# Adding the two halves of an attention chunk on VectorE instead of TensorE, with the mask pieces staged by ScalarE

## The chip, the cores and the metric

One core of one Trainium2 chip runs the kernel. The metric is the time of one execution on the device, in microseconds (us). Kernels are compared by the median of several runs; the profile shows one execution.

## What is computed

Attention with a bucket mask, followed by two MoE-like layers. The change touches attention alone. Its reference, cut to what matters (2 batches x 8 heads, 768 rows, head width 64, 6 bits):

```python
q_bits = (np.einsum('bhsd,dk->bhsk', q, proj) > 0)
k_bits = (np.einsum('bhsd,dk->bhsk', k, proj) > 0)
mask = q_bucket[:, :, :, None] == k_bucket[:, :, None, :]   # bucket = the 6 bits as a number
scores = scale * np.matmul(q, k.transpose(0, 1, 3, 2))
scores = np.where(mask, scores, -1000000000.0)
attn = np.exp(scores - max); attn = attn / (sum + 1e-09)
out = np.matmul(attn, v)
```

The result is laid out as 1536 rows of 512 and goes through relu(x w_in)^2 w_out and then through a routed layer of 8 experts.

## The kernel before

The 16 heads are worked in 8 pairs (`pair`, once for the first, a loop over six, once for the last). A pair has 12 tiles of 128 query rows by 768 keys, tt = 0 to 11, six for each head; three tiles make a chunk, so a pair has four chunks c = 0 to 3. Every engine has its own instruction queue, written out by hand in the order given here, and semaphores join them.

TensorE (`pair`, L1419 ff.) does for each tile tt, in this order: the scores of tile tt+2 (`scores`, L1373: four matmuls, 512 and 256 columns of each of two stacked operands; the mask rows are part of the operands); the first three transposes of the probabilities of tile tt (`turn_probs`, L1392, ring of three PSUM units); four products with v (`times_v`, L1406 and L1407, 384 columns each, into the PSUM bank PV); the other three transposes. Where tt-4 is a multiple of 3, all six transposes come ahead of the products, and the products start a new chunk. Beside the scores of tiles 2, 3, 5, 6, 8, 9 (MASK_TILES) a sixth of the next pair's mask is computed (L1324); beside those of tiles 10, 1, 4, 7 (BACK_TILES) a finished chunk is turned back (`turn_back`, L1355).

v is split into a rounded part and its remainder, side by side in 128 columns, so PV holds two halves of 64 partitions whose sum is the chunk's result, turned. ScalarE copies all 128 partitions to oT (`keep_oT`, L687), and TensorE multiplies oT with `fold`, two unit matrices of 64 on top of each other, which adds the halves and turns them back:

```python
for j in range(CHUNK_TILES):
    last_mm = mm(beside(z, CHUNK_TILES * HD)[:, HD * j:HD * j + HD], oT[c % 2][:, P * j:P * j + P],
                 fold, start=True, stop=True)
```

Each of these float32 matmuls shows as two matmul records and two weight loads.

ScalarE does for each tile tt: the exp with its row sums (`exp`, L667, two records), then for tile tt-1 the rounding of two units to pt_hi (`round_units`, L678), and where tt-7 is a multiple of 3 the copy to oT. The first rounding of a chunk and the copy wait for the end of an earlier chunk's products (pv_done).

VectorE does for each tile tt: for tile tt+1 the staging of a mask piece (`stage_mask`, L910 and L912, PSUM to mask_st, only for MASK_TILES), the scaling of a turned chunk into x_rows (`keep_x`, L955, only for BACK_TILES) and the maximum (L930); for tile tt-1 the two remainders pt_lo (`rest_units`, L939, which free a PSUM unit). Pieces 0 to 2 are 1 where the count of equal bits is the full one (popc), pieces 3 to 5 are -BIG where it is less.

GpSimd splits q, k and v of the next pair, and copies mask_st to the stacked operands (`place_masks`, through `copied`, L520). SyncE issues the loads. The waits that matter for the change:

```python
pe.wait_ge(oT_done, i * CHUNKS_PER_PAIR + c)                # times_v, first part of a chunk: PV is free
pe.wait_ge(oT_done, i * CHUNKS_PER_PAIR + (c + 1))          # turn_back
pe.wait_ge(exp_done, i * TILES_PER_PAIR + (tt - 1))         # scores
```

Of the kernel before, what the change touches and what calls it, by code (L numbers as in the profile page):

```python
# [5 lines left out]
F32 = mybir.dt.float32  # L6
# [4 lines left out]
ALU = mybir.AluOpType  # L11
# [57 lines left out]
def program(nc, qT, kT, v, proj_blocks, patterns, w_in, w_out, sb_rows, mod_id, mod_bias, w_gate, w1, w2,  # L69
            consts, tri, out):  # L70
    y_rows = nc.dram_tensor("y_rows", (TOK, DM), F32).ap()
    with ExitStack() as ctx:
# [33 lines left out]
        mb_sb = sb("mb_sb", [P, 2, NE], F32)  # L106
        oT = [sb(f"oT{c}", [P, CHUNK], F32) for c in range(2)]
        row_sum = sb("row_sum", [P, CHUNKS_PER_PAIR, CHUNK_TILES, 2], F32)
        row_eps = sb("row_eps", [P, CHUNKS_PER_PAIR, CHUNK_TILES], F32)
        row_inv = sb("row_inv", [P, CHUNKS_PER_PAIR, CHUNK_TILES], F32)  # L110
        x_rows = sb("x_rows", [P, PAIRS, QT, 2 * HD], F32)
        after_x = place[0]
# [186 lines left out]
        qk_split = sem("qk_split")  # L299
        masks_turned = sem("masks_turned")  # L300
        masks_staged = sem("masks_staged")
        masks_in = sem("masks_in")
# [207 lines left out]
        def _(pool):  # L510
# [33 lines left out]
            def place_masks(i, z):  # L544

                pool.wait_ge(masks_staged, i * MASK_UNITS + MASK_UNITS)
                pool.wait_ge(scores_done, i * TILES_PER_PAIR + (QT * (z + 1) - TILES_PER_PAIR))
                m = half(z, True)
                for c, stack in ((0, qb), (1, kb)):
                    copied(stack[z][m, :], mask_st[m, c, :], 1.0, masks_in, i * 4 + (2 * z + c + 1))  # L550

# [99 lines left out]
        def _(act):  # L651
# [29 lines left out]

            def keep_oT(i, c, first):
                act.wait_ge(pv_done, i * CHUNKS_PER_PAIR + (c + 1))
                if not (first and c < 2):

                    act.wait_ge(x_done, i * CHUNKS_PER_PAIR + (c - 1))
                nc.scalar.activation(oT[c % 2][:, :], ps[:, PV, 0:CHUNK], ACT.Copy).then_inc(oT_done, 1)  # L687

            def pair(i, first, last):
                for tt in range(TILES_PER_PAIR):  # L690
                    exp(i, tt, first)
                    if tt > 0:
                        round_units(i, tt - 1, first)
                    elif not first:
                        round_units(i - 1, TILES_PER_PAIR - 1, False)
                    c, r = divmod(tt - 7, CHUNK_TILES)
                    if r == 0:
                        if c >= 0:
                            keep_oT(i, c, first)
                        elif not first:  # L700
                            keep_oT(i - 1, c + CHUNKS_PER_PAIR, False)

            pair(0, True, False)
            with act.Fori(1, PAIRS - 1) as i:
# [10 lines left out]
            round_units(PAIRS - 1, TILES_PER_PAIR - 1, False)  # L715
            keep_oT(PAIRS - 1, 2, False)
            for t in range(1, 4):
                round_xt(t)
            keep_oT(PAIRS - 1, 3, False)

# [173 lines left out]
        def _(v_):  # L894
            v_.wait_ge(const_in, 16 * 7)
            nc.vector.memset(row_sum[:, :, :, 1], 1e-9).then_inc(eps_known, 1)
            v_.wait_ge(eps_known, 1)
# [7 lines left out]

            def stage_mask(m, part, dst, src):

                col = MASK_W * (m % 3)
                if m < 3:
                    return nc.vector.tensor_scalar(dst[part, col:col + MASK_W], src[part, :], popc[part, :], None,  # L910
                                                   ALU.is_equal)
                return nc.vector.tensor_scalar(dst[part, col:col + MASK_W], src[part, :], popc[part, :], -BIG,  # L912
                                               ALU.is_lt, ALU.mult)

            def tile_max(i, tt, first, last):

                z = tt % 2
                v_.wait_ge(scores_done, i * TILES_PER_PAIR + (tt + 1))
                if tt in MASK_TILES and not last:

                    v_.wait_ge(masks_in, i * 4 + 4)
                    m = MASK_TILES.index(tt)
                    stage_mask(m, slice(0, P), mask_st[:, m // 3, :], beside(z, MASK_W)).then_inc(masks_staged, 1)
                if tt in BACK_TILES:
                    c = BACK_TILES.index(tt)
                    if c == 0:
                        keep_x(i, c, z)
                    elif not first:
                        keep_x(i - 1, c, z)
                nc.vector.tensor_reduce(neg_max[:, z:z + 1], score_bank(z), AX, ALU.max,  # L930
                                        negate=True).then_inc(max_done, 1)

            def rest_units(i, tt):

                c, j = divmod(tt, CHUNK_TILES)
                for h in range(2):
                    v_.wait_ge(hi_done, i * (2 * TILES_PER_PAIR) + (2 * tt + h + 1))
# [22 lines left out]
            def pair(i, first, last_):  # L960
                for tt in range(TILES_PER_PAIR):
# [4 lines left out]
                    if tt > 0:  # L966
                        rest_units(i, tt - 1)
                    elif not first:
                        rest_units(i - 1, TILES_PER_PAIR - 1)

# [14 lines left out]
            for c, stack in ((0, qb), (1, kb)):  # L985
# [3 lines left out]
                for z in range(2):  # L989
                    for m in units:  # L990
                        v_.wait_ge(masks_turned, m + 1)
                        placed = stage_mask(m, half(z, True), stack[z], first_mask(m))
                        if z == 1:
# [24 lines left out]
            last_rows(1)  # L1018
            invert(PAIRS - 1, 3)
            for t in range(1, 4):  # L1020
                rest_xt(t)
            last_rows(2)
            last_rows(3)
# [295 lines left out]
        def _(pe):  # L1319
# [31 lines left out]
            def turn_back(i, c, z):  # L1351

                pe.wait_ge(oT_done, i * CHUNKS_PER_PAIR + (c + 1))
                for j in range(CHUNK_TILES):
                    last_mm = mm(beside(z, CHUNK_TILES * HD)[:, HD * j:HD * j + HD], oT[c % 2][:, P * j:P * j + P],  # L1355
                                 fold, start=True, stop=True)
                return last_mm

            def scores(i, tt, first, last):
# [11 lines left out]
                for a, b, start in ((qa[z], ka[z], True), (qb[z], kb[z], False)):  # L1371
                    for lo, hi in ((0, 512), (512, SEQ)):
                        last_mm = mm(bank[:, lo:hi], a[:, P * j:P * j + P], b[:, lo:hi], start=start, stop=not start)  # L1373
                if tt in MASK_TILES and not last:
# [75 lines left out]

            end = PAIRS - 1
            turn_back(end, 1, 1).then_inc(back_done, 1)
            times_v(end, 2, 2, False)
# [6 lines left out]

            pe.wait_ge(x_done, end * CHUNKS_PER_PAIR + 2)
            turn_back(end, 2, 1).then_inc(back_done, 1)

# [19 lines left out]
            def beside_first_step(f):  # L1483

                if f == 0:

                    pe.wait_ge(x_done, PAIRS * CHUNKS_PER_PAIR - 1)
                    turn_back(PAIRS - 1, 3, 1).then_inc(back_done, 1)
                if f == 1:
# [303 lines left out]
```

## Time and profile before

| | us |
|---|---|
| median of 3 runs | 732.97 (732.0 to 734.8) |
| the profiled execution | 731.03 |
| its span, first to last instruction | 729.2 |
| attention, within the span | to about 266 |
| TensorE busy | 704.5 |
| VectorE busy | 428.0 |
| ScalarE busy | 321.6 |
| GpSimd busy | 266.8 |

The span is what the trace covers; 1.8 us of the execution lie around it. PE is TensorE's matmuls, PEld its weight loads, which run beside the matmuls; DVE is VectorE, ACT ScalarE, POOL GpSimd. Matmuls are pipelined, so durations of neighbours overlap, and the pace of a group is read from the starts. The span divides into projections and first masks (to 33 us), attention, the first layer and the routed layer.

### The profile page before, as it was taken

To read this page: it belongs to the slowest core of one execution; us is meant where nothing else is said; L and a number is where in the kernel's file an instruction comes from. 1 tells how busy PE (TensorE), PEld (TensorE's weight loads), DVE (VectorE), ACT (ScalarE), POOL (GpSimd) and SP (SyncE) were. 2 spreads that over 40 slices of the span, in tenths; PEclk is the share of its full clock that TensorE was granted. 3 is DMA by queue.
4 is the path that set the end of the run, shared out by engine and by line. 5 is a ranking of instruction groups with operands and counts; after the bars stand their busy time and mean duration, and the time that the engine had idled before them with its cause. 6 is when DMAs were issued, how large, how long until landed. Compare 5 with 4: busy or idle time off the path is not lost.

```text
span 729.2 us, 12070 instructions
## 1 busy us (share of the span) xinstructions
PE 704.5 (97%) x3810; PEld 587.8 (81%) x3810; DVE 428.0 (59%) x825; ACT 321.6 (44%) x634; POOL 266.8 (37%) x271
## 2 busy tenths in 40 slices
PE   7799999999999999999999999999999899999994
PEld 3389999999999987888888888888885688877883
DVE  0589999999999956548555643564197611333110
ACT  0078878788787854221222221123144223443221
POOL 0666777677667751007004500720001222121111
PEclk9989999999999999999999999999999999999999
DMA  9921321321233030001100300001135541001011
GB/s 296 264 59 55 105 55 55 97 65 54 80 81 117 1 116 0 1 2 58 58 1 0 115 0 0 1 8 51 58 132 183 190 161 59 29 30 45 32 56 47
DMA packets 22508, 51.32 MB, mean 70 GB/s; under 512 B 3168, under 2 KB 5344, under 8 KB 22464
## 3 DMA queue, kind: packets, MB, share of 16 engines
q1 hardware_dynamic: 19008, 42.34, 18.3%
q0 software_dynamic: 2480, 7.87, 3.3%
q10 hardware_dynamic: 976, 0.56, 0.3%
q8 instruction: 23, 0.38, 0.2%
q14 instruction: 21, 0.17, 0.1%
HBM read 44.47 MB, written 6.55 MB: 70 GB/s over the span
## 4 chain that ended last, share of the span: by engine, by line
PE 89%; DVE 4%; DMA 2%; ACT 1%; issue 1%; SPq 1%; ACTq 0%; POOL 0%; POOLq 0%; DVEq 0%
PE ps L1373 9%; PE ps L1392 9%; PE ps L1576 6%; PE ps L1578 6%; PE ps L1577 6%; PE ps L1540 6%; PE ps L1542 6%; PE ps L1541 6%; PE ps L1406 5%; PE ps L1407 5%; PE ps L1661 3%; PE ps L1663 3%; PE ps L1662 3%; PE ps L1631 3%; PE ps L1633 3%; PE ps L1632 3%
## 5 line engine op out<-in xcount | busy, mean ns | idle before, releaser
L678 ACT ACTIVATE pt_hi<-ps 128x384 fp32r<-128x384 f32 x192 | 88.0, 499 | 42.1 <-PE ps L1392 26.9
L939 DVE TENSOR_TENSOR pt_lo<-ps,pt_hi 128x384 fp32r<-128x384 f32 x192 | 100.1, 551 | 10.4 <-ACT pt_hi L678 6.3
L731 ACT ACTIVATE relu<-ps 128x512 f32<-128x512 f32 x48 | 28.7, 598 | 175.6 <-PE ps L1542 175.6
L667 ACT ACTIVATE probs<-ps,neg_max 128x768 f32<-128x768 f32 x96 | 87.3, 909 | 26.0 <-DVE neg_max L930 25.9
L1392 PE MATMUL ps<-cst,probs 128*128 128x128 f32 x576 | 90.7, 275 | 0.9 <-DVE pt_lo L939 0.9
L930 DVE TENSOR_REDUCE neg_max<-ps 128x1 f32<-128x768 f32 x96 | 90.9, 946 | 0.0
L1117 DVE TENSOR_TENSOR sq<-relu 128x512 f32<-128x512 f32 x48 | 36.4, 759 | 71.6 <-ACT relu L731 71.2
L1540 PE MATMUL ps<-xt_hi,wi_hi 128*128 128x512 f32 x192 | 75.8, 395 | 0.0
L1576 PE MATMUL ps<-wo_hi,g_hi 128*128 128x512 f32 x192 | 74.9, 390 | 0.6 <-DVE xt_lo L1007 0.6
L1392 PEld LDWEIGHTS ps<-cst,probs 128*128 128x128 f32 x576 | 70.6, 145 | 5.9 <-DVE pt_lo L939 1.6
L1542 PE MATMUL ps<-xt_hi,wi_lo 128*128 128x512 f32 x192 | 74.8, 390 | 0.0
L1541 PE MATMUL ps<-xt_lo,wi_hi 128*128 128x512 f32 x192 | 74.7, 389 | 0.0
L1578 PE MATMUL ps<-wo_hi,g_lo 128*128 128x512 f32 x192 | 74.7, 389 | 0.0
L1577 PE MATMUL ps<-wo_lo,g_hi 128*128 128x512 f32 x192 | 74.7, 389 | 0.0
L1406 PE MATMUL ps<-pt_hi,vs 128*128 128x384 f32 x192 | 72.7, 379 | 0.0
L1407 PE MATMUL ps<-pt_lo,vs 128*128 128x384 f32 x192 | 64.7, 337 | 0.0
L520 POOL TENSOR_SCALAR wi_hi<-wi_raw 128x512 fp32r<-128x512 f32 x16 | 10.0, 622 | 143.3 <-PE ps L1542 140.5
L1154 DVE TENSOR_TENSOR y_acc<-ps,y_acc 128x512 f32<-128x512 f32 x48 | 32.4, 691 | 50.1 <-PE ps L1578 50.1
L1373 PE MATMUL ps<-ka,qa 128*128 128x512 f32 x192 | 57.3, 380 | 2.3 <-ACT probs L667 1.2
L1373 PE MATMUL ps<-kb,qb 128*128 128x512 f32 x192 | 50.3, 344 | 0.0
L639 POOL DMA_INDIRECT out<-y_slot,put_now x13 | 13.3, 1023 | 99.6 <-ACT y_slot L826 99.6
L1191 DVE TENSOR_TENSOR hT_lo<-ps,hT_hi 128x512 fp32r<-128x512 f32 x24 | 15.5, 685 | 53.0 <-ACT hT_hi L818 52.9
(198 smaller groups left out, 1473.0 us busy)
## 6 DMA issues: line engine op xcount, KB each, us to landing
w_raw<-w SPq DMA_DIRECT2D x16, 512.0 KB, 6.8
raw_k<-kT SPq DMA_DIRECT2D x32, 192.0 KB, 3.3
raw_q<-qT SPq DMA_DIRECT2D x32, 192.0 KB, 3.6
wi_raw<-w_in SPq DMA_DIRECT2D x4, 1024.0 KB, 5.1
wo_raw<-w_out SPq DMA_DIRECT2D x4, 1024.0 KB, 5.1
pair_raw<-qT SPq DMA_DIRECT2D x8, 384.0 KB, 6.7
pair_raw<-kT SPq DMA_DIRECT2D x8, 384.0 KB, 13.6
raw_v<-v SPq DMA_DIRECT2D x16, 192.0 KB, 2.4
```

The costliest lines, as they stand in the source:

```text
L930: nc.vector.tensor_reduce(neg_max[:, z:z + 1], score_bank(z), AX, ALU.max, negate=True).then_inc(max_done, 1)
L939: nc.vector.tensor_tensor(pt_lo[c % 2][sl], unit(tt, h).rearrange("p (k q) -> p k q", k=3), pt_hi[c % 2][sl].bitcast(F32), ALU.subtract).t ...
L1373: last_mm = mm(bank[:, lo:hi], a[:, P * j:P * j + P], b[:, lo:hi], start=start, stop=not start)
L1392: last_mm = nc.tensor.transpose(unit(tt, h)[:, P * u:P * u + P], probs[tt % 2][:, P * kt:P * kt + P], ident)
L1406: mm(ps[:, PV, 0:CHUNK], vs[z][:, kt, :], pt_hi[c % 2][:, kt, :], start=(kt == 0), stop=False)
L1407: last_mm = mm(ps[:, PV, 0:CHUNK], vs[z][:, kt, :], pt_lo[c % 2][:, kt, :], start=False, stop=(kt == QT - 1))
L1540: mm(ps[:, f, :], wi_hi[:, k, cols], xt_hi[:, k, tok], start=(k == 0), stop=False)
L1541: mm(ps[:, f, :], wi_hi[:, k, cols], xt_lo[:, k, tok], start=False, stop=False)
L1542: last_mm = mm(ps[:, f, :], wi_lo[:, k, cols], xt_hi[:, k, tok], start=False, stop=(k == KT - 1))
L1576: mm(ps[:, 4 + t, :], g_hi[:, f, tile], wo_hi[:, f, :], start=(f == 0), stop=False)
L1577: mm(ps[:, 4 + t, :], g_hi[:, f, tile], wo_lo[:, f, :], start=False, stop=False)
L1578: last_mm = mm(ps[:, 4 + t, :], g_lo[:, f, tile], wo_hi[:, f, :], start=False, stop=(f == FT - 1))
```

## The change

ScalarE copies only the lower half of PV (`keep_half`); VectorE adds the upper half to it and writes a result of 64 partitions (`add_halves`), between the two remainders of a tile; oT_done is now VectorE's signal. `turn_back` becomes three plain transposes of 64 partitions, and its wait stands ahead of the last scores matmul of the tile. The mask pieces 0 to 5 of the pairs 1 to 7 are staged by ScalarE, ahead of the exp of the same tile, as Relu(x + 1 - popc) and Sign(popc - x); GpSimd's copy of pieces 3 to 5 multiplies with -BIG. The first pair's masks stay on VectorE.

```diff
-        oT = [sb(f"oT{c}", [P, CHUNK], F32) for c in range(2)]
+        oT_hi = sb("oT_hi", [HD, CHUNK], F32)
+        oT = [sb(f"oT{c}", [HD, CHUNK], F32) for c in range(2)]
...
@@ place_masks (GpSimd)
-                for c, stack in ((0, qb), (1, kb)):
-                    copied(stack[z][m, :], mask_st[m, c, :], 1.0, masks_in, i * 4 + (2 * z + c + 1))
+                for c, stack, scale in ((0, qb, 1.0), (1, kb, -BIG)):
+                    copied(stack[z][m, :], mask_st[m, c, :], scale, masks_in, i * 4 + (2 * z + c + 1))
@@ ScalarE
-            def keep_oT(i, c, first):
+            def keep_half(i, c):
                 act.wait_ge(pv_done, i * CHUNKS_PER_PAIR + (c + 1))
-                if not (first and c < 2):
-
-                    act.wait_ge(x_done, i * CHUNKS_PER_PAIR + (c - 1))
-                nc.scalar.activation(oT[c % 2][:, :], ps[:, PV, 0:CHUNK], ACT.Copy).then_inc(oT_done, 1)
+                nc.scalar.activation(oT_hi[:, :], ps[0:HD, PV, 0:CHUNK], ACT.Copy).then_inc(half_kept, 1)
+
+            def stage_mask(i, m, z):
+
+                act.wait_ge(masks_in, i * 4 + 4)
+                col = MASK_W * (m % 3)
+                dst = mask_st[:, m // 3, col:col + MASK_W]
+                if m < 3:
+                    staged = nc.scalar.activation(dst, beside(z, MASK_W), ACT.Relu, bias=popc_1[:, :])
+                else:
+                    staged = nc.scalar.activation(dst, beside(z, MASK_W), ACT.Sign, scale=-1.0, bias=popc)
+                staged.then_inc(masks_staged, 1)
 
             def pair(i, first, last):
                 for tt in range(TILES_PER_PAIR):
+                    if tt in MASK_TILES and not last:
+                        act.wait_ge(max_done, i * TILES_PER_PAIR + (tt + 1))
+                        stage_mask(i, MASK_TILES.index(tt), tt % 2)
                     exp(i, tt, first)
...
+            act.wait_ge(popc_known, 1)
@@ VectorE
+            nc.vector.tensor_scalar(popc_1[:, :], popc, -1.0, 1.0, ALU.mult, ALU.add).then_inc(popc_known, 1)
...
-                if tt in MASK_TILES and not last:
-
-                    v_.wait_ge(masks_in, i * 4 + 4)
-                    m = MASK_TILES.index(tt)
-                    stage_mask(m, slice(0, P), mask_st[:, m // 3, :], beside(z, MASK_W)).then_inc(masks_staged, 1)
...
+            def add_halves(i, c):
+                v_.wait_ge(half_kept, i * CHUNKS_PER_PAIR + (c + 1))
+                nc.vector.tensor_tensor(oT[c % 2][:, :], ps[HD:P, PV, 0:CHUNK], oT_hi[:, :],
+                                        ALU.add).then_inc(oT_done, 1)
...
                     if tt > 0:
-                        rest_units(i, tt - 1)
+                        rest_units(i, tt - 1, (0,))
                     elif not first:
-                        rest_units(i - 1, TILES_PER_PAIR - 1)
+                        rest_units(i - 1, TILES_PER_PAIR - 1, (0,))
+                    c, r = divmod(tt - 7, CHUNK_TILES)
+                    if r == 0:
+                        if c >= 0:
+                            add_halves(i, c)
+                        elif not first:
+                            add_halves(i - 1, c + CHUNKS_PER_PAIR)
+                    if tt > 0:
+                        rest_units(i, tt - 1, (1,))
+                    elif not first:
+                        rest_units(i - 1, TILES_PER_PAIR - 1, (1,))
...
             invert(PAIRS - 1, 3)
+            add_halves(PAIRS - 1, 2)
             for t in range(1, 4):
                 rest_xt(t)
+            add_halves(PAIRS - 1, 3)
@@ TensorE
             def turn_back(i, c, z):
 
-                pe.wait_ge(oT_done, i * CHUNKS_PER_PAIR + (c + 1))
                 for j in range(CHUNK_TILES):
-                    last_mm = mm(beside(z, CHUNK_TILES * HD)[:, HD * j:HD * j + HD], oT[c % 2][:, P * j:P * j + P],
-                                 fold, start=True, stop=True)
+                    last_mm = nc.tensor.transpose(beside(z, CHUNK_TILES * HD)[:, HD * j:HD * j + HD],
+                                                  oT[c % 2][:, P * j:P * j + P], ident[0:HD, 0:HD])
...
                     for lo, hi in ((0, 512), (512, SEQ)):
+                        if tt in BACK_TILES and not start and hi == SEQ:
+                            c = BACK_TILES.index(tt)
+                            if c == 0:
+                                pe.wait_ge(oT_done, i * CHUNKS_PER_PAIR + 1)
+                            elif not first:
+                                pe.wait_ge(oT_done, i * CHUNKS_PER_PAIR + (c + 1 - CHUNKS_PER_PAIR))
```

The last pair's waits for its chunks 1, 2 and 3 (oT_done) are written out ahead of the three `turn_back` calls behind the loop.

## Rows read from the trace of the kernel before

**Rows 1.** The page, part 1: busy us, share of the span, instructions.

```profile
PE 704.5 (97%) x3810; PEld 587.8 (81%) x3810; DVE 428.0 (59%) x825; ACT 321.6 (44%) x634; POOL 266.8 (37%) x271
```

**Rows 2.** Busy time by stretch, 51 to 236 us: the engines, clock, DMA share, GB/s.

```profile
51.00:236.00 185.00, 185.00 (x1296) 168.36 (x1296) 174.16 (x353) 149.69 (x340) 131.18 (x130) 1.00 0.26 76
```

**Rows 3.** Waits of TensorE's weight loads, 51 to 236 us: total, times, longest.

```profile
PEld ps L1324 <- issue: 6.0, 38, 0.2
```

**Rows 4.** Timeline around one chunk's end: start, us, engine, what, count, idle before.

```profile
179.62 0.87 ACT L678 ACTIVATE pt_hi<-ps 128x384 fp32r<-128x384 f32 x2 [0.58 <-PE ps L1407]
180.14 1.02 DVE L939 TENSOR_TENSOR pt_lo<-ps,pt_hi 128x384 fp32r<-128x384 f32 x2
180.38 0.50 ACT L687 ACTIVATE oT<-ps 128x384 f32<-128x384 f32 x1
180.75 0.92 ACT L667 ACTIVATE probs<-ps,neg_max 128x768 f32<-128x768 f32 x1
181.05 0.19 PEld L1406 LDWEIGHTS ps<-pt_hi,vs 128*128 128x128 f32 x1
181.53 0.22 ACT L667 ACTIVATION_READ_ACCUMULATOR probs<-ps,neg_max 128x1 f32 x1
181.54 0.94 DVE L930 TENSOR_REDUCE neg_max<-ps 128x1 f32<-128x768 f32 x1
181.80 0.30 PEld L1373 LDWEIGHTS ps<-ka,qa 128*128 128x128 f32 x2
182.50 0.75 PEld L1355 LDWEIGHTS ps<-cst,oT 128*128 128x128 f32 x6
182.51 0.90 ACT L667 ACTIVATE probs<-ps,neg_max 128x768 f32<-128x768 f32 x1
183.12 0.37 PEld L1392 LDWEIGHTS ps<-cst,probs 128*128 128x128 f32 x3
183.45 0.19 PEld L1406 LDWEIGHTS ps<-pt_hi,vs 128*128 128x128 f32 x1
...
184.51 0.60 PE L1373 MATMUL ps<-ka,qa 128*128 128x512 f32 x2
```

**Rows 5.** Groups by line and shape, busy us, mean ns (L687: 51 to 236 us).

```profile
L910 DVE TENSOR_SCALAR mask_st<-ps,cst 128x256 bf16<-128x256 f32 x21 | 10.0, 475 | 2.4 <-PE ps L1324 2.4
L910 DVE TENSOR_SCALAR qb<-ps,cst 64x256 fp32r<-64x256 f32 x6 | 2.6, 480 | 0.5 <-PE ps L1324 0.5
L939 DVE TENSOR_TENSOR pt_lo<-ps,pt_hi 128x384 fp32r<-128x384 f32 x192 | 100.1, 551 | 10.4 <-ACT pt_hi L678 6.3
L955 DVE TENSOR_TENSOR x_rows<-ps,row_inv 128x192 f32 x24 | 8.6, 357 | 3.7 <-PE ps L1355 2.3
L1007 DVE TENSOR_TENSOR xt_lo<-ps,xt_hi 128x512 fp32r<-128x512 f32 x12 | 7.5, 681 | 0.9 <-ACT xt_hi L710 0.9
L687 ACT ACTIVATE oT<-ps 128x384 f32<-128x384 f32 x26 | 12.9, 497 | 0.0
L731 ACT ACTIVATE relu<-ps 128x512 f32<-128x512 f32 x48 | 28.7, 598 | 175.6 <-PE ps L1542 175.6
L667 ACT ACTIVATE probs<-ps,neg_max 128x768 f32<-128x768 f32 x96 | 87.3, 909 | 26.0 <-DVE neg_max L930 25.9
L738 ACT ACTIVATE gp<-sq,sb_sb 128x512 f32<-128x512 f32 x48 | 38.8, 809 | 2.3 <-DVE sq L1117 1.8
L667 ACT ACT_TABLE_LOAD x1 | 1.3, 1283 | 9.5 <-issue 9.5
```

**Rows 6.** Timeline at the end of attention: TensorE held by VectorE's remainder.

```profile
257.27 1.02 DVE L939 TENSOR_TENSOR pt_lo<-ps,pt_hi 128x384 fp32r<-128x384 f32 x2 [0.30 <-ACT pt_hi L678]
257.88 0.55 PE L1392 MATMUL ps<-cst,probs 128*128 128x128 f32 x3 [0.52 <-DVE pt_lo L939]
```

**Rows 7.** Timeline before a new pair: GpSimd's mask copies and the first scores.

```profile
197.61 0.83 POOL L520 TENSOR_SCALAR qb<-mask_st 64x768 fp32r<-64x768 bf16 x1 [0.30 <-POOL kb L540]
...
200.80 0.59 PE L1373 MATMUL ps<-ka,qa 128*128 128x512 f32 x2
```

More of the change, by code:

```diff
@@ L110, in program @@
         row_inv = sb("row_inv", [P, CHUNKS_PER_PAIR, CHUNK_TILES], F32)
+        popc_1 = sb("popc_1", [P, 1], F32)
         x_rows = sb("x_rows", [P, PAIRS, QT, 2 * HD], F32)
@@ L300, in program @@
         masks_turned = sem("masks_turned")
+        half_kept = sem("half_kept")
+        popc_known = sem("popc_known")
         masks_staged = sem("masks_staged")
@@ L698, in pair @@
                         if c >= 0:
-                            keep_oT(i, c, first)
+                            keep_half(i, c)
                         elif not first:
-                            keep_oT(i - 1, c + CHUNKS_PER_PAIR, False)
+                            keep_half(i - 1, c + CHUNKS_PER_PAIR)
+            act.wait_ge(popc_known, 1)
             pair(0, True, False)
@@ L715, in _ @@
             round_units(PAIRS - 1, TILES_PER_PAIR - 1, False)
-            keep_oT(PAIRS - 1, 2, False)
+            keep_half(PAIRS - 1, 2)
             for t in range(1, 4):
                 round_xt(t)
-            keep_oT(PAIRS - 1, 3, False)
+            keep_half(PAIRS - 1, 3)
             def quarter(q, first, last):
@@ L904, in keep_bits, with first_mask_rows @@
                                         ALU.is_gt).then_inc(bits_done, 1)
-            def stage_mask(m, part, dst, src):
+            def first_mask_rows(m, part, dst, src):
                 col = MASK_W * (m % 3)
@@ L931, in tile_max, with rest_units @@
                                         negate=True).then_inc(max_done, 1)
-            def rest_units(i, tt):
+            def add_halves(i, c):
+                v_.wait_ge(half_kept, i * CHUNKS_PER_PAIR + (c + 1))
+                nc.vector.tensor_tensor(oT[c % 2][:, :], ps[HD:P, PV, 0:CHUNK], oT_hi[:, :],
+                                        ALU.add).then_inc(oT_done, 1)
+            def rest_units(i, tt, halves=(0, 1)):
                 c, j = divmod(tt, CHUNK_TILES)
-                for h in range(2):
+                for h in halves:
                     v_.wait_ge(hi_done, i * (2 * TILES_PER_PAIR) + (2 * tt + h + 1))
@@ L991, in _ @@
                         v_.wait_ge(masks_turned, m + 1)
-                        placed = stage_mask(m, half(z, True), stack[z], first_mask(m))
+                        placed = first_mask_rows(m, half(z, True), stack[z], first_mask(m))
                         if z == 1:
@@ L1451, in _ @@
             end = PAIRS - 1
+            pe.wait_ge(oT_done, end * CHUNKS_PER_PAIR + 2)
             turn_back(end, 1, 1).then_inc(back_done, 1)
@@ L1461, in _ @@
             pe.wait_ge(x_done, end * CHUNKS_PER_PAIR + 2)
+            pe.wait_ge(oT_done, end * CHUNKS_PER_PAIR + 3)
             turn_back(end, 2, 1).then_inc(back_done, 1)
@@ L1487, in beside_first_step @@
                     pe.wait_ge(x_done, PAIRS * CHUNKS_PER_PAIR - 1)
+                    pe.wait_ge(oT_done, PAIRS * CHUNKS_PER_PAIR)
                     turn_back(PAIRS - 1, 3, 1).then_inc(back_done, 1)
```

## The prediction

> **What bounds the kernel now.** I read the page first, then the busy times of the attention loop by stretch, the waits of that stretch, the timeline of one chunk, and the groups by line for prices. The page has TensorE busy for 97% of the span [rows 1], which by itself proves little. The stretch from 51 to 236 us is the steady part of attention: TensorE is busy all of its 185.0 us at granted clock 1.00 (its upper level), VectorE 174.2, ScalarE 149.7 [rows 2]. The waits decide: there the only idle time of TensorE's weight loads is 0.2 us of "issue" before a mask matmul, 38 times; it waits for no other engine [rows 3]. So the time of attention is the length of TensorE's queue, and the change has to be read as what it takes from that queue and what waits it puts into it.
>
> A chunk (three tiles) lasts 7.1 us: 26 copies of oT in the 185.0 us [rows 2, 5]. The timeline of one shows how much room the queue has [rows 4]. ScalarE stands idle until the previous chunk's last product ends, then rounds two units (179.62), copies oT (180.38 to 180.88) and starts the exp (180.75), whose sum is read out by 181.75 (181.53 + 0.22). TensorE's queue reaches the first weights of the next chunk's products at 181.05. These products overwrite the bank that oT is copied from, and times_v waits for oT_done. The copy is 0.17 us early. The scores that need the exp load their weights at 181.80, only 0.05 after it. Both covers are thin.
>
> **The change, part by part.**
> *Turning back (L1355).* Six weight loads become three. They begin at 182.50, the next group at 183.12: 0.62 us for six. Three transposes of probs take 183.12 to 183.45, 0.11 each [rows 4]. A transpose of oT also loads 128 columns, so I take 0.33 for three and save 0.29 per chunk. Bounds: 0.10 each, the pace of the old loads (saves 0.31), and 0.12 (0.26); should its 64 moving columns alone set the pace it could be less, see the rivals. There are 32 chunks, all of them on TensorE's path: -9.3 us. The Trainium skill (TensorE: Matmul & The Clock Gate, Back-to-back issue gap) puts matmuls of 1 to 64 columns at a floor of some 25 ns each; three would then take 0.08 and the part would bring 17 us, and the same page's section on LDWEIGHTS instead charges the columns of the weights. The rows go with the latter.
>
> *The sum (add_halves).* It stands between ScalarE's copy and oT_done. The copy keeps its 384 elements per partition; halving the partitions does not shorten an instruction here: VectorE's mask op takes 480 ns on 64 partitions and 475 on 128 [rows 5]. So keep_half ends at 180.88 as oT did. VectorE's first half of the rests has begun at 180.14 and ends at 180.69, so it is free, and starts the add some 0.03 later (ScalarE's pt_hi of 179.62 ends at 180.12, the rest starts at 180.14). The trace has no such add. The nearest is the rest, also PSUM and SBUF in, 384 elements: 551 ns. Bounds: 357 (192 elements) and 681 (512 elements) [rows 5]; I take 0.55. VectorE to TensorE: a rest that starts at 257.27 ends at 257.82, and the transpose held by it starts at 257.88 [rows 6], so 0.05. Sum: 180.88 + 0.03 + 0.55 + 0.05 = 181.51, where TensorE was at 181.05. It stands still for 0.46 us (0.27 to 0.59 by the bounds), and everything behind it in its queue shifts. The wait of times_v is passed in 31 of 32 chunks, the first has none: +14.3 us (8.4 to 18.3).
>
> *What is queued behind the add.* The rest of the second half starts 0.47 after the add has started, near 181.39, not 180.61. It frees unit (tile, 1), which TensorE needs two groups of transposes later, at 183.12 + 0.46. The maximum after it goes from 181.54 to about 181.9, with the mask op of 0.47 gone from between [rows 5]. Its cover is the exp that before began at 182.51 [rows 4]. Cost nothing, while TensorE is late itself.
>
> *Masks on ScalarE.* 42 ops of VectorE go (7 pairs of 6 pieces), none on the path: no gain by themselves, while TensorE waits for nobody. ScalarE gets them, priced from its copies: 497 ns for 384 elements and 598 for 512, so about 0.40 for 256; the bias adds what exp has over a copy of 768, 909 - 800, so 0.51, and its successor starts 0.13 before its end, as the exp does after oT: 0.38. Bounds: 0.27 (no charge for the bias) and 0.68 (the 809 of the affine op with 512) [rows 5]. In three chunks of four a piece (tiles 2, 5, 8) stands right behind keep_half, before the exp. That exp is then read out at 182.13 and TensorE could load at 182.18; it gets there at 181.80 + 0.46 = 182.26. Covered by 0.08, thanks to the new stall alone. If the stall were not there, this would cost 0.38. The pieces of tiles 3, 6, 9 move the exp of 182.51 to about 183.3 (maximum done at 182.9, piece 0.38), read out near 184.3; its scores come at 184.51 + 0.46 - 0.29 = 184.68. Covered. The piece of tile 9 ends two chunks (14.2 us) after the 183.4 at which that of tile 3 does, near 197.6, just as GpSimd begins its two mask copies of 0.83 (197.61 to about 199.6); the next pair's first scores are at 200.80 [rows 7], so more than 1 us of delay there costs nothing. The scale -BIG in that copy replaces 1.0. masks_in was waited for earlier by VectorE, so its wait moved to ScalarE can't last longer.
>
> *Small edits.* The oT_done wait before a scores matmul comes 0.8 us after the sum; popc_1 is one tiny op, long before the first exp; the dropped x_done wait held nobody. No DMA changes; SP and GpSimd have the same queues. After the last pair the same order holds (two of the 32 chunks; one stall is counted), and the two MoE stages are untouched. At the start of attention, masks off VectorE may gain or lose a few tenths of a us.
>
> **The sum.** 31 x 0.46 - 32 x 0.29 = 14.3 - 9.3 = +5.0 us. The profiled execution took 731.03 (span 729.2 and 1.8 around it), so 736.0 on its own scale; the median of the runs shown is 732.97, 1.9 above, and by it 738.0.
>
> **The rivals.**
> *Break-even* (about 733, 729 to 736.5): the add near its lower bound, a stall of 0.27, gives 8.4 - 9.3 = -0.9; or the transposes run at some 0.05 each because only 64 rows are loaded, which saves 0.47 per chunk: 14.3 - 15.0 = -0.7. For it: the trace has neither form. Against: both are priced from neighbours with the same free size.
> *Faster, the wait is hidden* (723.7): TensorE's queue is 9.3 us shorter and the sum is ready by 181.05. This needs copy and add together in 0.17 us more than the copy alone has. Any VectorE op here on 192 elements already takes 0.36, so it would need work before times_v that the rows don't show, or a wait that is not where I put it. If VectorE rather than TensorE were the true bound (174.2 of 185.0), losing 42 ops of 0.47 would help too, but then the rows would have TensorE waiting.
> *Slower still, ScalarE decides* (742.6): the mask op with its 0.68 makes the exp ready at 182.48 instead of 182.26, 0.22 in 21 chunks, +4.6. It decides from a step of 0.46 on.
> *Table switches* (about 786): one table load of 1283 ns serves Exp, Copy, Relu and Identity, but no Sign is in the trace [rows 5]. If Sign needs another set, 21 pieces pay two loads each, 54 us, less some 6 of cover. The Trainium skill (ScalarE: Activation LUTs, Table sets: the hidden batching unit) says that cheap functions are in every set, though its examples don't name Sign; by its figure of about 2.7 us for a switch this case would cost twice that.
>
> **The chances.** The forecast 0.52, ScalarE decides 0.07, table switches 0.02, break-even 0.26, faster 0.13. About 0.5% (3.7 us) is what a measurement of this kernel can tell from no change. Slower by more: 0.60 (the low edge of the forecast's own range, +3, falls inside it); within: 0.27; faster: 0.13. The forecast's own range is 736 to 742; that for 8 in 10 takes in break-even and ScalarE: 730 to 744.
>
> **What would show it.** Right: the period of chunks grows from 7.1 to about 7.3 us; in 31 places TensorE waits 0.4 to 0.5 us before the first L1406 of a chunk, released by VectorE's add; the turned group lasts 0.33; VectorE is busy less, ScalarE more, near 165 of 185. Wrong: no such wait; scores held by the exp; transposes of oT far from 0.11; a second table load; an add far from 0.55.

## The result, and the profile after

The median of the changed kernel is 742.39 us (740.04 to 742.84, four runs), that of the kernel before 732.49 us (730.04 to 734.8, four runs). The ratio of the runs on record, which is not the quotient of the two medians, is 1.0124, 95% interval 1.0088 to 1.016. The change makes the kernel slower by 9.9 us; 738.0 was forecast, with 744 as the upper end. The profiled executions took 740.04 and 731.03 us, spans 738.2 and 729.2, so the traces hold 9.0 us of the 9.9.

First the profile's page, part 1, of the changed kernel (it answers to [rows 1]):

```profile
PE 703.9 (95%) x3714; PEld 575.7 (78%) x3714; DVE 429.2 (58%) x816; ACT 334.0 (45%) x676; POOL 266.4 (36%) x271
```

and the stretch from 51 to 236 us (as [rows 2]):

```profile
51.00:236.00 185.00, 179.14 (x1173) 153.24 (x1172) 166.29 (x328) 155.42 (x366) 126.25 (x124) 1.00 0.27 75
```

TensorE is no longer busy all the time: 5.9 us of the stretch are empty, at the same granted clock. ScalarE has gone up by 5.7, VectorE down by 7.9. The waits of the same stretch (engine, tile and line; what it waits for; total, times, longest) name the place. [Rows 3] had one line for the weight loads; the first two lines here are of that kind.

```profile
PEld ps L1383 <- issue: 6.2, 25, 0.3
PEld ps L1353 <- issue: 6.0, 38, 0.2
PEld ps L1440 <- DVE oT L947: 5.1, 12, 0.4
PEld ps L1440 <- issue: 3.4, 7, 0.5
PEld ps L1440 <- POOL vs L564: 2.9, 6, 0.5
```

The three lines of L1440 stand for one wait. The first weight load of a chunk's products (L1440) is put down to VectorE 12 times, to "issue" 7 times and to GpSimd 6 times: 25 chunks, 11.4 us, 0.46 each. The GpSimd operation named writes v into the buffer that the chunk just ended has left, for products two chunks later, so it isn't what these products wait for; the length and the place are those of the wait for VectorE, whose add ends 0.05 or 0.12 before the weights each time. One group did not exist before: 25 times 0.25 before the weights of turning back (L1383). The timeline of a chunk (start, us, engine, what; in brackets the idle time before and what ended it) answers to [rows 4]:

```profile
185.14 0.87 ACT L682 ACTIVATE pt_hi<-ps 128x384 fp32r<-128x384 f32 x2 [0.57 <-PE ps L1441]
185.89 0.10 PEld L1353 LDWEIGHTS ps<-bits,patt 96*128 x1 [0.16 <-issue]
185.90 0.48 ACT L688 ACTIVATE oT_hi<-ps 64x384 f32<-64x384 f32 x1
186.27 0.46 ACT L696 ACTIVATE mask_st<-ps,popc 128x256 bf16<-128x256 f32 x1
186.41 0.56 DVE L947 TENSOR_TENSOR oT<-ps,oT_hi 64x384 f32<-64x384 f32 x1 [0.19 <-ACT oT_hi L688]
186.63 0.89 ACT L671 ACTIVATE probs<-ps,neg_max 128x768 f32<-128x768 f32 x1
187.03 0.19 PEld L1440 LDWEIGHTS ps<-pt_hi,vs 128*128 128x128 f32 x1 [0.43 <-DVE oT L947]
187.66 0.36 PEld L1407 LDWEIGHTS ps<-ka,qa 128*128 128x128 f32 x2
188.17 0.51 PE L1407 MATMUL ps<-kb,qb 128*128 128x512 f32 x2
188.61 0.26 PEld L1383 LDWEIGHTS ps<-cst,oT 64*128 64x128 f32 x3 [0.25 <-issue]
188.94 0.31 PEld L1426 LDWEIGHTS ps<-cst,probs 128*128 128x128 f32 x3
189.21 0.19 PEld L1440 LDWEIGHTS ps<-pt_hi,vs 128*128 128x128 f32 x1
```

The copy ends at 186.38, the add runs from 186.41 to 186.97, TensorE goes on at 187.03: the chain of the prediction, link by link. From the first copy (53.511) to the 30th (266.212) a chunk takes 7.334 us on average, before 7.051 (53.019 to 257.506): 29 x 0.283 = 8.2 of the 9.0 us. The first copy comes 0.5 later, and what follows the 30th takes 0.3 more. So 8.2 of the 9.0 us lie between these two copies. (The first copy of the kernels below comes at 53.0 to 55.1, so 0.5 there says nothing.) The groups by line (busy us, mean ns of one, idle before), for the prices:

```profile
L947 DVE TENSOR_TENSOR oT<-ps,oT_hi 64x384 f32<-64x384 f32 x32 | 17.9, 559 | 6.9 <-ACT oT_hi L688 6.9
L688 ACT ACTIVATE oT_hi<-ps 64x384 f32<-64x384 f32 x32 | 15.3, 479 | 2.4 <-PE ps L1441 2.4
L696 ACT ACTIVATE mask_st<-ps,popc 128x256 bf16<-128x256 f32 x21 | 9.8, 467 | 1.0 <-DVE neg_max L942 1.0
L671 ACT ACT_TABLE_LOAD x1 | 1.3, 1283 | 35.6 <-DVE neg_max L942 35.6
```

Sign brought no second table load.

### The profile page after: what moved, and what is told of

It reads as the page before. It is cut to its first block, busy times and chain, and to the rows that moved or that the text cites. A ratio compares the mean times of both kernels' runs of the same rounds, so it can differ in the third digit from the quotient of the medians.

```text
span 738.2 us, 11900 instructions
## 1 busy us (share of the span) xinstructions
PE 703.9 (95%) x3714; PEld 575.7 (78%) x3714; DVE 429.2 (58%) x816; ACT 334.0 (45%) x676; POOL 266.4 (36%) x271
## 4 chain that ended last, share of the span: by engine, by line
PE 82%; DVE 5%; ACT 4%; issue 4%; POOL 2%; DMA 2%; SPq 1%; ACTq 1%; POOLq 0%; DVEq 0%
PE ps L1407 6%; PE ps L1613 6%; PE ps L1615 6%; PE ps L1614 6%; PE ps L1577 6%; PE ps L1579 6%; PE ps L1578 6%; PE ps L1440 6%; PE ps L1426 5%; PE ps L1441 5%; PE ps L1698 3%; PE ps L1700 3%; PE ps L1699 3%; PE ps L1668 3%; PE ps L1670 3%
## 5 line engine op out<-in xcount | busy, mean ns | idle before, releaser
L956 DVE TENSOR_TENSOR pt_lo<-ps,pt_hi 128x384 fp32r<-128x384 f32 x192 | 103.5, 554 | 17.1 <-ACT pt_hi L682 14.5
L1440 PE MATMUL ps<-pt_hi,vs 128*128 128x384 f32 x192 | 72.8, 379 | 7.7 <-DVE oT L947 5.4
L1426 PEld LDWEIGHTS ps<-cst,probs 128*128 128x128 f32 x576 | 69.0, 142 | 7.0 <-DVE pt_lo L956 0.8
L1407 PE MATMUL ps<-ka,qa 128*128 128x512 f32 x192 | 55.0, 368 | 4.7 <-ACT probs L671 3.6
L643 POOL DMA_INDIRECT out<-y_slot,put_now x13 | 13.3, 1021 | 100.5 <-ACT y_slot L842 100.5
L1440 PEld LDWEIGHTS ps<-pt_hi,vs 128*128 128x128 f32 x192 | 36.2, 188 | 14.6 <-issue 6.5
```

The source lines that it names most:

```text
L956: nc.vector.tensor_tensor(pt_lo[c % 2][sl], unit(tt, h).rearrange("p (k q) -> p k q", k=3), pt_hi[c % 2][sl].bitcast(F32), ALU.subtract).t ...
L1426: last_mm = nc.tensor.transpose(unit(tt, h)[:, P * u:P * u + P], probs[tt % 2][:, P * kt:P * kt + P], ident)
L1440: mm(ps[:, PV, 0:CHUNK], vs[z][:, kt, :], pt_hi[c % 2][:, kt, :], start=(kt == 0), stop=False)
```

## The experiments

Two questions were put. Where do the 4 us come from that the forecast lacks, and which of the three parts (turning back, the wait for the sum, the mask pieces) carries what? "Chunk" is the mean of 25 distances between copies in the middle of attention (from the second copy to the 27th) in each profiled execution. Each ratio compares a kernel with runs of the kernel before that were made along with it; their medians are 731.9 (e1, e2, e4, e5), 732.42 (e6 to e9) and 732.57 (e10). Apart from e1 the ratios stay within 2% of 1, so it is by their intervals and by the chunks that they are told apart.

| kernel | median us | ratio to before, 95% | chunk us |
|---|---|---|---|
| before | 732.49 | | 7.075 |
| the change | 742.39 | 1.0124 (1.0088 to 1.016) | 7.354 |
| change, turned by f32 matmuls (e1) | 758.56 | 1.0355 (1.0306 to 1.0403) | 7.841 |
| before, three transposes of 64 rows (e2) | 729.03 | 0.9949 (0.9921 to 0.9978) | 6.926 |
| before, mask pieces on ScalarE (e4) | 742.38 | 1.014 (1.008 to 1.02) | 7.334 |
| change, mask pieces on VectorE (e5) | 741.26 | 1.0126 (1.0074 to 1.0177) | 7.354 |
| change, copy between the roundings (e6) | 739.63 | 1.0109 (1.0058 to 1.0159) | 7.250 |
| e6, mask pieces on VectorE (e9) | 738.60 | 1.008 (1.0056 to 1.0104) | 7.216 |
| e6, four buffers pt_hi (e7) | 727.03 | 0.9907 (0.9875 to 0.9939) | 6.833 |
| before, four buffers pt_hi (e8) | 729.80 | 0.9957 (0.9931 to 0.9983) | 6.983 |
| e7, mask pieces on VectorE (e10) | 732.57 | 1.0 (0.9976 to 1.0024) | 7.107 |

**Turning back as before.** The changed kernel, with each transpose replaced by an ordinary f32 matmul of the same 64 rows, which leaves two records:

```diff
-last_mm = nc.tensor.transpose(beside(z, CHUNK_TILES * HD)[:, HD * j:HD * j + HD],
-                              oT[c % 2][:, P * j:P * j + P], ident[0:HD, 0:HD])
+last_mm = mm(beside(z, CHUNK_TILES * HD)[:, HD * j:HD * j + HD], oT[c % 2][:, P * j:P * j + P],
+             ident[0:HD, 0:HD], start=True, stop=True)
```

> The changed kernel with its new sum and masks, but turned back by plain float32 matmuls as before (six records of 64 rows instead of three transposes). Theory (the loss is TensorE's wait for VectorE's sum, 0.46 us in c = 0 and 2 and 0.52 in c = 1 and 3, 31 times, less what the transposes save): the wait stays as it is and the saving is gone, so before + 15 us, about 748; if loads of 64 rows cost 0.1 us per chunk by themselves, as the 0.09 us gap ahead of the first transpose in the changed kernel suggests, before + 18, about 751. Rival (the transposes save nothing, since their loads of 64 rows drain the array): 742, as the changed kernel.

758.56, above either expectation. So six records of 64 rows are dearer than six of 128, and the timeline after the last scores matmuls shows where:

```profile
181.33 0.51 PE L1407 MATMUL ps<-kb,qb 128*128 128x512 f32 x2
181.77 0.74 PEld L1383 LDWEIGHTS ps<-cst,oT 64*128 64x128 f32 x6 [0.25 <-issue]
182.57 0.31 PEld L1426 LDWEIGHTS ps<-cst,probs 128*128 128x128 f32 x3
182.85 0.19 PEld L1440 LDWEIGHTS ps<-pt_hi,vs 128*128 128x128 f32 x1
```

The kernel before has this row in the timeline of [rows 4]:

```profile
182.26 0.51 PE L1373 MATMUL ps<-kb,qb 128*128 128x512 f32 x2
```

From the start of the last two scores matmuls to the weights of the products it is 182.85 - 181.33 = 1.52 here and 183.45 - 182.26 = 1.19 before: as many records, 0.33 more. One by one, the first weights start 0.21 after the start of the last matmul ahead of them (0.003 in the kernel before), the six follow each other by 0.11 as before, and the next group's start 0.26 after the sixth (0.06 before): 0.20 more at either end, of which 0.06 is regained behind. Against the change itself (189.21 - 188.17 = 1.04) it is 0.48 more, and the chunk is longer by just that (7.841 - 7.354 = 0.49).

**Turning back alone.** The kernel before, with `oT_done` waits placed as in the change and three transposes of the lower 64 partitions of oT. It leaves out the upper half of the result; add and copy are as before.

```diff
-                pe.wait_ge(oT_done, i * CHUNKS_PER_PAIR + (c + 1))
                 for j in range(CHUNK_TILES):
-                    last_mm = mm(beside(z, CHUNK_TILES * HD)[:, HD * j:HD * j + HD], oT[c % 2][:, P * j:P * j + P],
-                                 fold, start=True, stop=True)
+                    last_mm = nc.tensor.transpose(beside(z, CHUNK_TILES * HD)[:, HD * j:HD * j + HD],
+                                                  oT[c % 2][0:HD, P * j:P * j + P], ident[0:HD, 0:HD])
```

> The kernel before with only TensorE's part of the change: three transposes of the lower 64 partitions of oT, with the waits placed as in the change; the upper half of each chunk is left out of the result. No new wait. The prediction's term: 32 x 0.29 = 9.3 us less, 723. Theory after the trace of the changed kernel (last scores matmul to next transposes 0.73 before, 0.54 after): 32 x 0.20 = 6.3 less, 726. Rival (nothing saved in a queue that is held elsewhere): 732.

729.03, 2.9 below the 731.9 of before beside it, where the forecast's term was 9.3. The chunk falls by 7.075 - 6.926 = 0.149, not 0.29. Its timeline shows where the rest stays:

```profile
180.30 0.51 PE L1378 MATMUL ps<-kb,qb 128*128 128x512 f32 x2
180.74 0.26 PEld L1354 LDWEIGHTS ps<-cst,oT 64*128 64x128 f32 x3 [0.25 <-issue]
181.06 0.31 PEld L1397 LDWEIGHTS ps<-cst,probs 128*128 128x128 f32 x3
181.34 0.19 PEld L1411 LDWEIGHTS ps<-pt_hi,vs 128*128 128x128 f32 x1
```

From the first of the three loads to the next group it takes 0.32 (181.06 - 180.74) in place of 0.62: in sum the price of the prediction. But they begin 0.44 after the kb matmuls, and the six of before 0.24 after them (182.50 - 182.26): 0.20 given back in front, listed as "issue". Behind, probs to products takes 0.28 and not 0.33: 0.05 regained. -0.30 + 0.20 - 0.05 = -0.15.

The 0.32 is right by luck. The prediction had three steps of 0.11. A window narrowed to the third load of the change shows it 0.12 after the first, which starts at 188.61:

```profile
188.73 0.14 PEld L1383 LDWEIGHTS ps<-cst,oT 64*128 64x128 f32 x1
```

So the loads follow each other by 0.06 and the next group comes 0.21 after the third; over the chunks of the change and of e2 the steps are 0.056 to 0.065 and 0.204 to 0.209. Transposes of 64 rows are cheap inside their group, as the break-even rival had them, and dear at both of its edges. It is not the new place of the wait that makes the late start: the weights of the last three groups of the change, which have their wait directly ahead, start 0.20 to 0.32 after the start of the last matmul, those of the kernel before in the same three places 0.001 to 0.003.

**Mask pieces alone.** The kernel before, with the six pieces of a pair on ScalarE as in the change:

```diff
             def pair(i, first, last):
                 for tt in range(TILES_PER_PAIR):
+                    if tt in MASK_TILES and not last:
+                        act.wait_ge(max_done, i * TILES_PER_PAIR + (tt + 1))
+                        stage_mask(i, MASK_TILES.index(tt), tt % 2)
                     exp(i, tt, first)
```

> The kernel before with only the mask pieces moved to ScalarE. Theory: the exp behind a copy and a piece is ready 0.37 us later than before, where the scores had 0.05 to 0.1 us of cover, so TensorE is held some 0.3 us in 21 chunks, before the scores matmuls: +6 us, 739. Rival (the relief of VectorE is worth something, 42 x 0.41 us): at or below 732.

742.38. Its chunks with a piece behind the copy take 7.47, 7.47 and 7.35 us where before has 7.115, 7.115 and 6.98, and the one without stays at 7.10: 0.36 in 21 places, 7.5 us. (Its profiled execution is some 4.5 us longer behind the 30th copy than that of before, e1's 6; from 500 to 600 us both have a granted clock of 0.97 where before has 1.00. So the pieces are read from the chunks and not from the time as a whole.) The timeline of such a chunk, with the wait in brackets:

```profile
172.06 0.50 ACT L689 ACTIVATE oT<-ps 128x384 f32<-128x384 f32 x1
172.43 0.49 ACT L699 ACTIVATE mask_st<-ps,cst 128x256 bf16<-128x256 f32 x1
172.79 0.92 ACT L669 ACTIVATE probs<-ps,neg_max 128x768 f32<-128x768 f32 x1
173.57 0.23 ACT L669 ACTIVATION_READ_ACCUMULATOR probs<-ps,neg_max 128x1 f32 x1
173.85 0.30 PEld L1386 LDWEIGHTS ps<-ka,qa 128*128 128x128 f32 x2 [0.48 <-ACT probs L669]
```

The piece pushes the exp back by its step of 0.36, and the scores' weights come 0.05 after its read-out.

**Mask pieces back.** The same edit the other way round, in the changed kernel: the loop of ScalarE without the three lines, and VectorE's `tile_max` with its piece as before.

> The changed kernel with the mask pieces staged by VectorE again. Theory (pieces on ScalarE are covered by TensorE's wait for the sum): 742, within 1 us of the changed kernel. Rival (ScalarE's pieces are part of the loss of 9 us): 738 or less.

741.26, and the chunk is 7.354 as in the change to the last digit. While TensorE is held by the sum, the pieces cost nothing on ScalarE and bring nothing on VectorE. With e4 this shows two waits that cover each other: either alone lengthens a chunk (by 0.43 the one, in three of four chunks by 0.36 the other), and both together cost no more than the one.

**Order of the copy.** In the change, `keep_half` was put between ScalarE's two roundings of a tile, so that the sum is begun earlier:

```diff
                     nc.scalar.activation(pt_hi[c % 2][:, 3 * h:3 * h + 3, P * j:P * j + P],
...
+                    if h == 0 and between:
+                        between()
```

> The changed kernel with one order changed on ScalarE: the copy of the half between the two roundings instead of behind them. The sum is then ready near 2.1 us after the chunk's last product instead of 2.37 (the add can start when VectorE's first remainder is under way). Theory (two waits cover each other: the wait for the sum, and the exp behind the mask piece, ready at 2.93, whose scores would now come at 2.7): chunks without a piece get 0.29 us shorter, the others nothing, since the exp takes over: mean chunk 7.28, total 739 to 741. Rival (the wait for the sum is the whole loss): all chunks 0.29 shorter, 733.

> The same order, with the mask pieces staged by VectorE again (exp ready at 2.56). Theory: both waits are gone from the same chunks: every chunk 0.2 to 0.29 us shorter than in the changed kernel (mean 7.07 to 7.15, as the kernel before has 7.08), total 731 to 735. Rival (pieces on VectorE delay its add and the maximum, so that the wait for the sum stays): 7.25 and more, 739.

739.63 and 738.60; the chunk gained 0.10 and 0.14, and the expectation for e9 (731 to 735) missed. The timeline of e6 shows why so little came:

```profile
176.18 0.49 ACT L682 ACTIVATE pt_hi<-ps 128x384 fp32r<-128x384 f32 x1 [0.44 <-PE ps L1444]
176.57 0.47 ACT L690 ACTIVATE oT_hi<-ps 64x384 f32<-64x384 f32 x1
176.71 0.56 DVE L959 TENSOR_TENSOR pt_lo<-ps,pt_hi 128x384 fp32r<-128x384 f32 x1 [0.39 <-ACT pt_hi L682]
177.30 0.56 DVE L950 TENSOR_TENSOR oT<-ps,oT_hi 64x384 f32<-64x384 f32 x1
177.97 0.19 PEld L1443 LDWEIGHTS ps<-pt_hi,vs 128*128 128x128 f32 x1 [0.34 <-issue]
```

The copy starts 0.39 after the first rounding, where the change has 0.76, and ends at 177.04. But VectorE is in the first half of the remainder until 177.27, and the add begins at 177.30, 0.26 after the copy's end (0.25 to 0.33 in e9). From the first rounding to the add it is 1.12 in place of 1.27: 0.15 gained, of 0.37 that the copy gained. In the chunks with a piece the exp then takes over, as expected: the scores' weights come 0.05 after its read-out, 0.73 or 0.80 after the products' first weights in place of 0.64. In e9, where the pieces are back on VectorE, they come after 0.63 again, and the chunk is 0.03 shorter. What is late is the first rounding itself. It waits for the previous chunk's last product (the 0.44 in brackets), because two buffers `pt_hi` serve both.

**Four buffers.** So e7 takes away what makes that rounding wait. It has the order of e6, four `pt_hi`, and VectorE's first remainder of a chunk now waits for the products of two chunks back, since `pt_lo` stays at two:

```diff
-        pt_hi = [sb(f"pt_hi{c}", [P, QT, CHUNK], F32R) for c in range(2)]
+        pt_hi = [sb(f"pt_hi{c}", [P, QT, CHUNK], F32R) for c in range(4)]
...
-                if j == 0 and not (first and c < 2):
-                    act.wait_ge(pv_done, i * CHUNKS_PER_PAIR + (c - 1))
+                if j == 0 and not first:
+                    act.wait_ge(pv_done, i * CHUNKS_PER_PAIR + (c - 3))
...
+                if j == 0 and halves[0] == 0 and not (first and c < 2):
+                    v_.wait_ge(pv_done, i * CHUNKS_PER_PAIR + (c - 1))
```

> The changed kernel with four buffers of pt_hi instead of two and the copy between the roundings. The first rounding of a chunk no longer waits for the products of an older one, so copy, second rounding, mask piece and exp all come 0.3 to 0.4 us earlier. Theory: the sum is ready before TensorE gets to it (1.88 us after the last product) and the exp at about 2.57, scores at 2.6: no wait, chunks of 6.93 as in the run with the transposes alone, total 726 to 729, faster than both kernels. Rival (VectorE is now late: first remainder, add and maximum in a row): some wait of 0.1 to 0.3 stays, 730 to 737.

> Control: the kernel before with four buffers of pt_hi, nothing else. TensorE waits for nobody there, so no change is expected: 732, chunks of 7.08. Rival (the buffers bring time by themselves): below 729.

> Four buffers of pt_hi and the copy between the roundings, with the mask pieces staged by VectorE again. Theory (in the run with the pieces on ScalarE no wait of TensorE is left, so it can't get faster; VectorE gets 42 pieces of 0.41 us and its add back): chunks of 6.83 to 6.9, total 727 to 729, the same within what can be told. Rival (VectorE is then late with the add in the chunks with a piece, as it was in the run with the order alone, where the add started 0.27 to 0.31 after the copy): chunks near 7.0, total 731 and more; this would show that moving the pieces is what the new order needs.

e7 is 727.03, 0.9% below the kernel before by the ratio, and 2% below the change. Timeline of a chunk, then the stretch of [rows 2]:

```profile
136.39 0.49 ACT L681 ACTIVATE pt_hi<-ps 128x384 fp32r<-128x384 f32 x1
136.99 0.48 ACT L689 ACTIVATE oT_hi<-ps 64x384 f32<-64x384 f32 x1
137.67 0.56 DVE L949 TENSOR_TENSOR oT<-ps,oT_hi 64x384 f32<-64x384 f32 x1
138.50 0.19 PEld L1444 LDWEIGHTS ps<-pt_hi,vs 128*128 128x128 f32 x1
```

```profile
51.00:236.00 185.00, 185.00 (x1259) 164.49 (x1258) 178.28 (x352) 165.91 (x392) 136.57 (x134) 1.00 0.27 76
```

ScalarE rounds while the products still run, the sum ends at 138.23, and TensorE comes at 138.50, 0.27 later. In one chunk of four it comes 0.12 after the add, so there the room is used up. TensorE is busy for all of the 185.0 us again.

The control e8 has the buffers alone in the kernel before. It was expected at 732 and measured 729.8. By [rows 3] TensorE waited for nobody, so nothing was there to win; the chunk still fell by 0.09. (The profiled execution doesn't show it in its span, since its first copy comes 1.7 later.) The read-out of the exp and the scores' weights in e8:

```profile
139.35 0.19 PEld L1407 LDWEIGHTS ps<-pt_hi,vs 128*128 128x128 f32 x1
139.72 0.21 ACT L667 ACTIVATION_READ_ACCUMULATOR probs<-ps,neg_max 128x1 f32 x1
139.99 0.36 PEld L1374 LDWEIGHTS ps<-ka,qa 128*128 128x128 f32 x2
```

From the products' first weights to the scores' it is 139.99 - 139.35 = 0.64, as in the change (187.66 - 187.03 = 0.63), in e7 and in e10, so this is the pace of the queue. In [rows 4] it is 181.80 - 181.05 = 0.75, and the weights come 0.05 after the exp's read-out, the time of a hand-over between engines here, and so in every chunk. That was a wait, of 0.11. It was not listed: the weight loads stand idle for 0.11 there, less than the view of waits took up in [rows 3], and TensorE's matmuls show no idle time at all. In e8 three chunks of four are rid of it, the fourth still has 0.75. What it is worth is less than 0.11: without it the time from the scores' weights to those of turning back is 0.75 and not 0.69, so 0.07 per chunk is won where it is gone, 0.05 on average.

A second wait is gone with it. The fourth of the six transposes ahead of a chunk's products needs a unit that VectorE's remainder frees. In the kernel before (windows narrowed to the one remainder and the one load):

```profile
144.69 0.56 DVE L939 TENSOR_TENSOR pt_lo<-ps,pt_hi 128x384 fp32r<-128x384 f32 x1 [0.39 <-ACT pt_hi L678]
145.30 0.14 PEld L1392 LDWEIGHTS ps<-cst,probs 128*128 128x128 f32 x1
```

The remainder ends at 145.25 and the weights start at 145.30, 0.27 after the third's; in e8 it is 0.11. That is the one chunk of four that has no mask piece ahead, and from the first of the six to the products' weights it takes 0.78 there, in e8 0.66: 0.03 on average. In the other three the weights follow the remainder by the same 0.05, but only 0.15 after the third's, and the products lose nothing by it. The two waits make 0.08 of the 0.09.

e10 came out at 732.57, as the rival had it. Timeline:

```profile
167.00 0.47 DVE L928 TENSOR_SCALAR mask_st<-ps,cst 128x256 bf16<-128x256 f32 x1
167.39 0.94 DVE L945 TENSOR_REDUCE neg_max<-ps 128x1 f32<-128x768 f32 x1
167.64 0.48 ACT L689 ACTIVATE oT_hi<-ps 64x384 f32<-64x384 f32 x1
168.26 0.54 DVE L961 TENSOR_TENSOR pt_lo<-ps,pt_hi 128x384 fp32r<-128x384 f32 x1
168.83 0.56 DVE L950 TENSOR_TENSOR oT<-ps,oT_hi 64x384 f32<-64x384 f32 x1
169.44 0.19 PEld L1445 LDWEIGHTS ps<-pt_hi,vs 128*128 128x128 f32 x1 [0.27 <-DVE oT L950]
```

The copy ends at 168.12, but VectorE is behind by its mask piece and adds from 168.83, 0.71 later (0.49 to 0.78 over the chunks). With the sum begun this early, taking the pieces off VectorE is worth 7.107 - 6.833 = 0.27 per chunk, where in the change as made it is worth nothing (e5).

Not tried: adding both halves straight from the accumulator bank without a copy, a transpose that loads all 128 rows, and the four buffers in the change without the new order of the copy.

## Why the prediction was right, and where it was not

- **TensorE waits for the sum: right.** Forecast 0.03 to start, 0.55 for the add, 0.05 to TensorE; measured 0.032, 0.559 and 0.053 in half of the chunks, 0.116 in the others (in those GpSimd works on v at the same time; what the further 0.06 is was not settled). The first weights come 2.335 or 2.397 us after the start of the last product, before 1.88: a stall of 0.49 on average, forecast 0.46.
- **"It waits for no other engine": the statement failed.** e8 shows a wait of 0.11 for the exp and one for VectorE's remainder. The prediction saw the 0.05 behind the exp and called it a thin cover. It was a wait already, and the new stall swallows it, so that a chunk grows by 7.354 - 6.926 = 0.43 and not by 0.49: the products' weights come 0.49 later, the scores' follow them by 0.64 and not 0.76, and the part up to turning back gives 0.06 of that back. 31 x 0.43 = 13.3, forecast 14.3.
- **"Save 0.29 per chunk": this is the term that was mis-sized.** The step that failed is the price taken from transposes of 128 rows: three times 0.11, and nothing for what lies on either side of the group. Measured are 0.06 from load to load, 0.21 from the third to the next group and 0.20 of late start; the first two add up to the forecast's 0.33 by luck, the late start was missing. e2 shows 0.149, and e8 to e7 again 0.150, with the sum covered there. 32 x 0.149 = 4.8, forecast 9.3, outside the bounds of 0.26 and 0.31. Both bounds came from loads of 128 rows, so they bounded nothing here. [Rows 3] had the hint: the one idle time of the weight loads, up to 0.2 of "issue" 38 times, stands before the mask weights, and those have 96 rows (in the timeline of the change at 185.89).
- **The sum.** 13.3 - 4.8 = +8.5 of the +9.0 between the traces; the rest was not followed. Forecast +5.0.
- **Masks covered: right, with its condition.** e5 finds no cost in the change, e4 finds 0.36 where the prediction said that it would cost 0.38 without the stall. The cover was as thin as said: exp ended 2.92 after the last product's start, weights 2.97. The price of a piece was 0.467 long and 0.37 in step (forecast 0.51 and 0.38). ScalarE was not near 165 of 185 us busy, as the sign had it, but 155.4: the pieces add 17.8 in the stretch, and with longer chunks less of the other work falls into it.
- **Rivals.** The table switch is excluded by the single load. "The wait is hidden" did not occur in the change; e7 shows what it needed: ScalarE's first rounding out of the way of the products. "ScalarE decides" gave almost the measured time (742.6), but by a mechanism that e5 refutes. Break-even needed a short add, which 559 ns excludes, or transposes at 0.05 each. They do follow each other by 0.06, so its premise nearly held; the joins took back what it would have brought.

## What to carry to other kernels

Work taken from a full engine and put into another engine's chain is paid by the chain's slack at that place, here 0.17 us against an added 0.6; find the slack first, and make it (here with two more buffers and the copy between the roundings, 727.03 against 742.39) before the work is moved. A weight load on the critical engine that begins one hand-over (0.05) after another engine's end in every chunk was waiting for it here, though the view of waits had no row of it; what such a wait is worth is read from the chunk (0.05) and not from the load's delay (0.11). When an edit changes an instruction's shape, price also its join with the instructions on either side; a group's mean step, taken up to the next group, hides it.

## What the runs showed of the hardware

- Weights of 64 rows between weights of 128 rows start about 0.2 us later after a matmul than weights of 128 do (0.44 against 0.24 after the start of the last two scores matmuls), in e1, e2, e7 and the change alike, and the weights of 128 rows behind them are late too (0.21 after the third transpose's, 0.26 after the sixth record's in e1, against 0.06 in the kernel before). Six records of 64 rows cost 0.33 more than six of 128. Weights and moving operand change their rows together in these runs, so which of the two counts was not told apart. The 96-row mask weights have an idle time of the same kind; that it is the number of rows there too was not tried by itself. By the Trainium skill (TensorE: Matmul & The Clock Gate, the section LDWEIGHTS) the columns alone set the time of a load. The six f32 records of e1 agree, 0.11 apart with 64 rows as with 128; the three transposes, 0.06 apart with the same 128 columns, do not, and the joins, where the number of rows changes, aren't in that rule.
- Three transposes with 64 rows of weights and 64 moving columns follow each other by 0.06 us, f32 matmul records of the same shape by 0.11 (e1).
- An add of 64 partitions with 384 elements each takes 559 ns on VectorE, a remainder of 128 partitions 554: half the partitions save nothing.
- Two waits of weight loads for other engines were worth some 0.08 us per chunk together while TensorE showed 185.0 busy of 185.0 us [rows 2] (e8).
